# A chunked delta-rule attention with two dense blocks behind it: the 16 by 16 blocks inverted by 8 by 8 halves, and the key-scale steps split between odd and even chunks

## The chip, the core and the metric

The kernel runs on one core of one Trainium2 chip. The core has TensorE (PE, matmuls; PEld are its weight loads), VectorE (DVE), ScalarE (ACT), GpSimd (POOL) and SyncE (SP), which only issues transfers. Each engine works through its own list of instructions in order and waits on semaphores for the others. The metric is the device time in microseconds (us) of one execution; lower is better.

## The reference, cut to what matters

Inputs are q, k and v of shape (4, 8, 768, 48) and beta of shape (4, 8, 768), all float32. For each of the 32 pairs of batch and head:

```python
k_n = k / (np.linalg.norm(k, axis=-1, keepdims=True) + 1e-06)
for t in range(S):                       # S = 768
    y[t] = q[t] @ state                  # state is 48 x 48, zero at the start
    v_old = k_n[t] @ state
    state = state + beta[t] * outer(k_n[t], v[t] - v_old)
```

The result goes as x of shape (4, 768, 384) through two dense blocks: a Fourier transform over tokens and features, a layer norm and an MLP; then a gate by cosine and sine of x @ w_theta, a mix over tokens and one more layer. The change doesn't touch them.

## The kernel before

**Chunks.** The 768 steps are cut into 12 chunks of C = 64 tokens, numbered c = 0 to 11. Partitions hold two sets of 64 tokens (batches in halves), so NG = 16 groups stand beside each other on the free axis. Within a chunk the sequential rule is a triangular system. Its strictly triangular matrix comes from key products (`gram`). Its four 16 by 16 diagonal blocks (BLK = 16) are inverted exactly by DVE, all 128 of them at once, one a partition. What is left between the blocks is applied by three more matrix steps on PE (`hop` 1 to 3).

**What each engine does in iteration c.** All five engines run a loop `for c in range(-3, 12)`; the negative ones fill the pipeline.

- PE: `predicted(c)` (L360, keys times state), `corner(c, 0)` and `corner(c, 1)` (L305, operands TT and AP), `solve(c)` (L305, Yv and TT), `gram(c+2)` in two parts (L337), `hop` 1, 2, 3 (L305, Yv and ET), `turn(c+3)` (L325) before hop 3, `queried` (L394), `grow` (L420), `direct` (L305, Yv and AP).
- ACT copies what PE leaves in its banks: Yv after `solve` and after each hop (`copied_y(c, 0..3)`), AP after `gram`, KQ after `turn`, the state Sv, TT, the output Yo. It also makes the upper part of the diagonal blocks (Dy), and in odd iterations the square root of the key norms (`root`, nr<-nr). All of these are recorded as L443.
- DVE: `make_x(c)` (L672, Yv, v minus what the state predicts), `mask_e` (L660, ET), then for the next chunk `eliminate` (L630 and L633), `scaled_u` (L643, Ux) and `blocks_out` (L652, To, a transpose). Then, in odd iterations, `norm` (L563, sums of squared keys for a pair of chunks), and in even iterations `scale` (L576 to L589, eleven small steps that turn the norms into 1/norm and beta/norm²; ms and cT are results). Then `blocks_in(c+2)` (L603 Dy, L607 Tt, L614 Rb, L616 Ti, L618 and L620 U in bank 3).
- POOL: in odd iterations `squares` (L270, kk), then `scaled_v(c+1)` (L278, Vv by ms) and `mask_p(c+2)` (L290, AP). SP issues the loads of k, q and v.

**The inversion.** For a column j = 1 to 14 `eliminate` makes an outer product of U[0:j, j] and Ti[j, j+1:16] (L630) and subtracts it from U[0:j, j+1:16] (L633). Each of the 28 instructions waits for the one before. U lies in bank 3 (PSUM), Ti and prod in SBUF. ET, which `hop` 1 needs, and Yv, which `solve` needs, come before it in DVE's list.

**Order.** The lists are written out by hand as the loops have them. The semaphores that matter below: `solve` waits for both halves of Yv (s_xe) and for TT (s_tt); `corner` for TT and AP; `root` for both sums of its pair (s_n2) and for all steps of the pair before; `scale` for the root (s_sq); `blocks_in(n)` for the eleven steps of its pair (s_nr); `scaled_v` for the first five.

Of the kernel before, what the change touches and what calls it, by code (L numbers as in the profile page):

```python
# [8 lines left out]
ALU = mybir.AluOpType  # L9
ACT = mybir.ActivationFunctionType  # L10
AX = mybir.AxisListType
# [4 lines left out]
P = 128  # L16
# [11 lines left out]
BLK = 16  # L28
# [18 lines left out]
def constants():  # L47

    m, n = np.arange(HALF), np.arange(HALF + 1)
# [6 lines left out]
    d, k = np.arange(DM // 4 + 1), np.arange(DM // 4 + 1)  # L56
# [8 lines left out]
    p = np.arange(P)  # L65
    t, col = p % C, np.arange(C)
    mE = -1.0 * (t[:, None] // BLK < col[None, :] // BLK)
    mirrored = np.where(col == 0, 0, C - col)
    mP = 1.0 * np.stack([t[:, None] < col[None, :], t[:, None] < mirrored[None, :]], 1)
    upper = -1.0 * (np.arange(BLK)[:, None] < np.arange(BLK)[None, :])  # L70
    mU = np.broadcast_to(upper.reshape(1, BLK * BLK), (P, BLK * BLK))
# [15 lines left out]
def attention(nc, A, X, bank, block, sem, ident, preload, weights_ahead):  # L87
    with ExitStack() as ph:
        def sb(name, shape, dt=F32):
            return ph.enter_context(nc.sbuf_tensor(name, shape, dt))  # L90

        HG = NG // 2
        RK, RT, RA = 6, 4, 3
        half = (slice(0, C), slice(C, P))
        feat = (slice(0, D), slice(C, C + D))
# [24 lines left out]
        Rb = sb("Rb", [P, BLK, BLK])  # L120
        Ti = sb("Ti", [P, BLK, BLK])
        prod = sb("prod", [P, 56])
        Kb = sb("Kb", [P, RK, HG, 2, C])
        kk = sb("kk", [P, 2, NG, D])
        Vv = sb("Vv", [P, 2, NG, D])
        U = bank[3][:, 0:BLK * BLK].rearrange("p (k i) -> p k i", k=BLK)

        s_cst, s_id = sem("tables_loaded"), sem("identity_loaded")
# [20 lines left out]
        def there(n):  # L149
            return 0 <= n < NC  # L150
# [53 lines left out]

        STEPS = 2 + 28
        IN = 5
        NS = 11
# [233 lines left out]
        def _(act):  # L441
# [95 lines left out]
            for c in range(C0, NC):  # L537
                copied_y(c, 0)
                gram(c + 2, (0, 2))
                copied_y(c, 1)  # L540
                gram(c + 2, (1, 3))
                upper_blocks(c + 2)
                copied_y(c, 2)
                turned(c + 3)
                copied_y(c, 3)
                grown(c)
                placed(c + 1)
                output(c, 0)
                output(c, 1)
                if c % 2:  # L550
                    root((c + 3) // 2)
                store(c)

        @block.vector
        def _(dve):
# [8 lines left out]

            def scale(pair):
                if not 0 <= pair < NC // 2:
                    return
                dve.wait_ge(s_sq, pair + 1)
                if pair >= 2:
                    dve.wait_ge(s_vp, 2 * pair - 2)  # L570
                if pair >= 2:
                    dve.wait_ge(s_us, 2 * (2 * pair - 2))
# [18 lines left out]
                ]  # L591
                for i, step in enumerate(steps):
                    step().then_inc(s_nr, 1)
                    if i < NS - 1:
                        dve.wait_ge(s_nr, NS * pair + i + 1)

            def blocks_in(n):
# [17 lines left out]
                dve.wait_ge(s_in, at + 4)  # L615
                dve.tensor_tensor(Ti[:], Rb[:], by, ALU.mult).then_inc(s_in, 1)  # L616
                dve.wait_ge(s_in, at + 5)
                dve.tensor_tensor(bank[3][:, 0:BLK * BLK], Ti[:].rearrange("p j i -> p (j i)"), mU[:], ALU.mult).then_inc(s_iv, 1)  # L618
                dve.wait_ge(s_iv, STEPS * n + 1)
                dve.memset(bank[3][:, 0:BLK * BLK:BLK + 1], 1.0).then_inc(s_iv, 1)  # L620

            def eliminate(n, cols):
                if not there(n):
                    return
                for j in cols:
                    at = STEPS * n + 2 * j
                    m = BLK - 1 - j
# [1185 lines left out]
```

## Time and profile before

| | us |
|---|---|
| median of 3 runs | 832.17 |
| lowest, highest | 830.99, 832.19 |
| the profiled execution | 828.37 |
| its span | 826.6 |
| busy: PE, PEld | 776.2, 548.5 |
| busy: DVE, ACT, POOL | 517.9, 318.0, 164.7 |

The span is the stretch that the trace covers, from the first recorded work to the last; the 1.77 us between it and the time of the same execution lie around it. The profiled execution was 3.8 us faster than the median of the other runs, so sums made in the trace are compared with its own time and then carried over to the median. The attention part ends at 262.8 us of the span; the rest is the two dense blocks. A row of a timeline gives start, duration, engine, line, operation, the tiles out<-in with their shapes, the number of instructions, and in brackets the idle time before them with what ended it.

### The profile page before, as it was taken

The page shows a single profiled execution, that of the slowest core. Times are in us where ns is not written, and L with a number is a line of the kernel's source. Part 1 is how long each engine was busy: PE and PEld are TensorE (multiplying, and loading weights), DVE is VectorE, ACT ScalarE, POOL GpSimd, SP SyncE. Part 2 cuts the span into 40 slices and gives each one's busy share as a digit, 9 for nine tenths or more (in the row PEclk, how much of TensorE's full clock was granted, in tenths as well). Part 3 has the DMA queues.
Part 4 walks back from the last instruction along what each step waited for, and adds up shares of the span by engine and source line. Part 5 has one row for each costly group of instructions (what it writes and reads, how often), then busy time and mean ns, then how long its engine had stood idle before and what let it go on. Part 6 is the DMA issues. An engine that isn't in the chain of part 4 may idle for free.

```text
span 826.6 us, 24886 instructions
## 1 busy us (share of the span) xinstructions
PE 776.2 (94%) x10976; PEld 548.5 (66%) x10976; DVE 517.9 (63%) x1238; ACT 318.0 (38%) x635; POOL 164.7 (20%) x201
## 2 busy tenths in 40 slices
PE   4688888889889999999999999999999999999998
PEld 3687888888887556655665566666666666666664
DVE  4997889797847783724472346365646767767422
ACT  3465565655542350403140315142433434424211
POOL 2531423232200102200130010003213323224100
PEclk9899999999999999999999999999999999999999
DMA  9133343322121141010101001000000000000101
GB/s 210 41 92 82 94 110 91 90 71 62 42 80 42 58 131 41 12 47 1 41 18 58 1 29 29 1 1 1 1 1 1 11 20 20 36 14 20 39 28 50
DMA packets 45390, 37.54 MB, mean 45 GB/s; under 512 B 27425, under 2 KB 39651, under 8 KB 45283
## 3 DMA queue, kind: packets, MB, share of 16 engines
q1 hardware_dynamic: 38501, 30.90, 13.2%
q10 hardware_dynamic: 6781, 5.05, 2.5%
q8 instruction: 87, 1.43, 0.7%
q14 instruction: 21, 0.16, 0.1%
HBM read 26.50 MB, written 4.72 MB: 38 GB/s over the span
## 4 chain that ended last, share of the span: by engine, by line
PE 85%; DVE 5%; issue 4%; ACT 3%; DMA 2%; SPq 0%; POOL 0%; DVEq 0%; ACTq 0%
PE bank L305 15%; PE bank L1083 6%; PE bank L1131 6%; PE bank L1085 6%; PE bank L1130 6%; PE bank L1129 6%; PE bank L1084 6%; PE bank L1065 5%; PE bank L1067 5%; PE bank L1066 5%; PE bank L337 3%; PE bank L360 1%; ACT Dy L443 1%; PE bank L1107 1%; PE bank L1108 1%
## 5 line engine op out<-in xcount | busy, mean ns | idle before, releaser
L1248 ACT ACTIVATE hT_hi<-bank 128x384 f16<-128x384 f32 x96 | 46.7, 490 | 159.7 <-PE bank L1067 159.6
L1528 DVE SCALAR_TENSOR_TENSOR hT_lo<-bank,hT_hi 128x384 f16<-128x384 f32 x96 | 53.3, 556 | 73.3 <-ACT hT_hi L1248 72.5
L1065 PE MATMUL bank<-unT,wA 128*128 128x384 f16 x288 | 94.0, 326 | 0.3 <-DVE hT_lo L1528 0.3
L1083 PE MATMUL bank<-wA,hT_hi 128*128 128x384 f16 x288 | 93.9, 326 | 0.0
L1067 PE MATMUL bank<-unT,wA 128*128 128x384 f16 x288 | 93.9, 326 | 0.0
L1085 PE MATMUL bank<-wA,hT_lo 128*128 128x384 f16 x288 | 93.9, 326 | 0.0
L1066 PE MATMUL bank<-unT,wA 128*128 128x384 f16 x288 | 93.9, 326 | 0.0
L1084 PE MATMUL bank<-wA,hT_hi 128*128 128x384 f16 x288 | 93.9, 326 | 0.0
L305 PE MATMUL bank<-Yv,ET 64*64 64x48 f32 x2304 | 75.4, 218 | 4.2 <-ACT Yv L443 2.3
L305 PEld LDWEIGHTS bank<-Yv,ET 64*64 64x64 f32 x2304 | 72.9, 135 | 7.1 <-ACT Yv L443 4.5
L443 ACT ACTIVATE Yv<-bank,rows 128x384 f32<-128x384 f32 x72 | 40.6, 578 | 65.6 <-PE bank L305 65.4
L290 POOL TENSOR_TENSOR AP<-AP,mP 128x256 f32<-128x256 f32 x48 | 33.9, 728 | 141.4 <-ACT AP L443 132.1
L1536 DVE SCALAR_TENSOR_TENSOR X<-bank,X 128x384 f32<-128x384 f32 x24 | 13.4, 557 | 73.4 <-PE bank L1085 73.4
L955 POOL TENSOR_SCALAR fourier_temps<-fourier_temps 128x384 f32<-128x384 f32 x24 | 20.1, 837 | 153.2 <-DVE fourier_temps L1563 153.2
L1129 PE MATMUL bank<-wt_hi,z_first 128*128 128x384 f16 x144 | 46.9, 326 | 0.0
L1130 PE MATMUL bank<-wt_lo,z_first 128*128 128x384 f16 x144 | 46.9, 326 | 0.0
L1131 PE MATMUL bank<-wt_hi,z_first 128*128 128x384 f16 x144 | 46.9, 326 | 0.0
L1129 PE MATMUL bank<-wt_hi,wA 128*128 128x384 f16 x144 | 46.9, 326 | 0.0
L1130 PE MATMUL bank<-wt_lo,wA 128*128 128x384 f16 x144 | 46.9, 326 | 0.0
L1131 PE MATMUL bank<-wt_hi,wA 128*128 128x384 f16 x144 | 46.9, 326 | 0.0
L1065 PEld LDWEIGHTS bank<-unT,wA 128*128 128x128 f16 x288 | 28.2, 98 | 20.7 <-issue 1.8
L1066 PEld LDWEIGHTS bank<-unT,wA 128*128 128x128 f16 x288 | 28.2, 98 | 18.7 <-issue 1.1
(212 smaller groups left out, 1660.5 us busy)
## 6 DMA issues: line engine op xcount, KB each, us to landing
Kb<-k_dram SPq DMA_DIRECT2D x24, 192.0 KB, 3.6
Vv<-v_dram SPq DMA_DIRECT2D x12, 384.0 KB, 4.0
z_first<-w_dram SPq DMA_DIRECT2D x8, 576.0 KB, 4.0
z_first<-wt_dram SPq DMA_DIRECT2D x8, 576.0 KB, 3.6
out_dram<-hT_hi SPq DMA_DIRECT2D x24, 192.0 KB, 1.9
KQ<-q_dram SPq DMA_DIRECT2D x44, 96.0 KB, 2.3
X<-Yo ACTq DMA_DIRECT2D x12, 192.0 KB
X<-Yo ACTq DMA_DIRECT2D x10, 189.0 KB
```

Of the source, the lines that this page charges most:

```text
L305: mm = pe.matmul(out[half[h]], a[half[h]], b[half[h]], start=first, stop=last, skip_group_check=True)
L443: return nc.scalar.activation(out, in_, func, scale=scale)
L1065: pe.matmul(out, w1[0][:, k, cols], unT[0][:, k, :], start=(k == 0), stop=False)
L1066: pe.matmul(out, w1[0][:, k, cols], unT[1][:, k, :], start=False, stop=False)
L1067: mm = pe.matmul(out, w1[1][:, k, cols], unT[0][:, k, :], start=False, stop=(k == KD - 1))
L1083: pe.matmul(out, hT[0][:, f, cols], w2[0][:, f, :], start=(f == 0), stop=False)
L1084: pe.matmul(out, hT[0][:, f, cols], w2[1][:, f, :], start=False, stop=False)
L1085: mm = pe.matmul(out, hT[1][:, f, cols], w2[0][:, f, :], start=False, stop=(f == KF - 1))
L1129: pe.matmul(out, zh, wt[0][:, c, t, cols], start=first, stop=False)
L1130: pe.matmul(out, zh, wt[1][:, c, t, cols], start=False, stop=False)
L1131: mm = pe.matmul(out, zl, wt[0][:, c, t, cols], start=False, stop=last)
L1528: dve.scalar_tensor_tensor(hT[1][:, f, :], bank[3 + m % 3][:, 0:TG * P], 0.0, hT[0][:, f, :], ALU.max, ALU.subtract).then_inc(s_hl, 1)
```

## The change

The elimination now runs on the two 8 by 8 diagonal halves of each block at once, for columns 1 to 6 only, with a fourth axis of 2 in each access. The upper right 8 by 8 corner is then made by `corner_block`: a product of 512 elements (U's upper left half with Ti's corner), a sum over 8, a product of 512 with U's lower right half, and a sum over 8. Ti is now the negated block, so that its sign fits both. Of the eleven steps of `scale`, from pair 2 on the first five stand at the end of the odd iteration before, and the last six where all eleven stood. For this, in odd iterations from 1 on, `norm` moves up between the elimination and `corner_block`, and `root` on ACT moves from behind the output copies to ahead of `copied_y(c, 3)`. In iterations -3 to 0 the old places are kept.

```diff
-    upper = -1.0 * (np.arange(BLK)[:, None] < np.arange(BLK)[None, :])
+    upper = 1.0 * (np.arange(BLK)[:, None] < np.arange(BLK)[None, :])
...
+        def both_diagonal(padded):
+            t = padded.rearrange("p (b w) -> p b w", b=2)[:, :, 0:HB * BLK]
+            return t.rearrange("p b (k i) -> p b k i", k=HB)[:, :, :, 0:HB]
+
+        Ud, Td = both_diagonal(bank[3][:, 0:BLK * BLK + BLK]), both_diagonal(Ti_padded[:])
...
-        STEPS = 2 + 28
+        STEPS = 2 + 2 * (HB - 2) + 4
...
                 turned(c + 3)
+                if c % 2 and c > -1:
+                    root((c + 3) // 2)
                 copied_y(c, 3)
...
-                if c % 2:
+                if c in (-3, -1):
                     root((c + 3) // 2)
...
-                dve.wait_ge(s_sq, pair + 1)
-                if pair >= 2:
-                    dve.wait_ge(s_vp, 2 * pair - 2)
-                if pair >= 2:
+                if 0 in part:
+                    dve.wait_ge(s_sq, pair + 1)
+                    if pair >= 2:
+                        dve.wait_ge(s_vp, 2 * pair - 2)
+                elif pair >= 2:
                     dve.wait_ge(s_us, 2 * (2 * pair - 2))
...
-                dve.tensor_tensor(Ti[:], Rb[:], by, ALU.mult).then_inc(s_in, 1)
+                dve.scalar_tensor_tensor(Ti, Rb[:], -1.0, by, ALU.mult, ALU.mult).then_inc(s_in, 1)
...
-                    pr = prod[:, 0:j * m].rearrange("p (k i) -> p k i", k=j)
-                    dve.tensor_tensor(pr, U[:, 0:j, j:j + 1].broadcast_to([P, j, m]),
-                                      Ti[:, j:j + 1, j + 1:BLK].broadcast_to([P, j, m]), ALU.mult).then_inc(s_iv, 1)
+                    pr = prod[:, 0:2 * j * m].rearrange("p (b k i) -> p b k i", b=2, k=j)
+                    dve.tensor_tensor(pr, Ud[:, :, 0:j, j:j + 1].broadcast_to([P, 2, j, m]),
+                                      Td[:, :, j:j + 1, j + 1:HB].broadcast_to([P, 2, j, m]), ALU.mult).then_inc(s_iv, 1)
                     dve.wait_ge(s_iv, at + 1)
-                    dve.tensor_tensor(U[:, 0:j, j + 1:BLK], U[:, 0:j, j + 1:BLK], pr, ALU.subtract).then_inc(s_iv, 1)
+                    dve.tensor_tensor(Ud[:, :, 0:j, j + 1:HB], Ud[:, :, 0:j, j + 1:HB], pr, ALU.add).then_inc(s_iv, 1)
+
+            def corner_block(n):
...
+                dve.tensor_tensor(pr, U[:, 0:HB, 0:HB].unsqueeze(2).broadcast_to([P, HB, HB, HB]),
+                                  Ti[:, 0:HB, HB:BLK].rearrange("p l i -> p i l").unsqueeze(1).broadcast_to([P, HB, HB, HB]),
+                                  ALU.mult).then_inc(s_iv, 1)
+                dve.wait_ge(s_iv, at + 1)
+                dve.tensor_reduce(Xb[:], pr, AX.X, ALU.add).then_inc(s_iv, 1)
+                dve.wait_ge(s_iv, at + 2)
+                dve.tensor_tensor(pr, Xb[:].unsqueeze(2).broadcast_to([P, HB, HB, HB]),
+                                  U[:, HB:BLK, HB:BLK].rearrange("p l i -> p i l").unsqueeze(1).broadcast_to([P, HB, HB, HB]),
+                                  ALU.mult).then_inc(s_iv, 1)
+                dve.wait_ge(s_iv, at + 3)
+                dve.tensor_reduce(U[:, 0:HB, HB:BLK], pr, AX.X, ALU.add).then_inc(s_iv, 1)
...
-                eliminate(c + 1, (1, 2, 3, 4, 5, 6, 7, 8, 9, 10, 11, 12, 13, 14))
+                eliminate(c + 1, (1, 2, 3, 4, 5, 6))
+                if c % 2 and c > -1:
+                    norm((c + 3) // 2)
+                corner_block(c + 1)
                 scaled_u(c + 1)
                 blocks_out(c + 1)
-                if c % 2:
+                if c in (-3, -1):
                     norm((c + 3) // 2)
-                else:
-                    scale((c + 2) // 2)
+                elif c in (-2, 0):
+                    scale((c + 2) // 2, range(5))
+                if c % 2 and c > -1:
+                    scale((c + 3) // 2, range(5))
+                elif c % 2 == 0:
+                    scale((c + 2) // 2, range(5, NS))
                 blocks_in(c + 2)
```

On DVE, in the odd iteration 1, this is what stood between the last step of the elimination and the Yv of the next chunk before the change:

```order
L633 TENSOR_TENSOR bank<-bank,prod 128x14
L643 SCALAR_TENSOR_TENSOR Ux<-bank,rows,cT 128x16x16 x2
L652 STREAM_TRANSPOSE To<-Ux 128x16x32
L563 TENSOR_REDUCE nr<-kk 128x16 x2
L603 SCALAR_TENSOR_TENSOR Dy<-AP,rows,Dy 128x256 x2
L607 STREAM_TRANSPOSE Tt<-Dy 128x512
```

And this is what stands there now, from the last step of the shorter elimination on (prod and Xb are scratch tiles, bank is bank 3 with U in it):

```order
L645 TENSOR_TENSOR bank<-bank,prod 128x2x6
L574 TENSOR_REDUCE nr<-kk 128x16 x2
L653 TENSOR_TENSOR prod<-bank,Ti 128x512
L657 TENSOR_REDUCE Xb<-prod 128x64
L659 TENSOR_TENSOR prod<-Xb,bank 128x512
L663 TENSOR_REDUCE bank<-prod 128x8x8
L673 SCALAR_TENSOR_TENSOR Ux<-bank,rows,cT 128x16x16 x2
L682 STREAM_TRANSPOSE To<-Ux 128x16x32
L588 TENSOR_SCALAR nr<-nr 128x32
L589 RECIPROCAL nr<-nr 128x32
L590 TENSOR_TENSOR nr<-nr 128x32
L591 TENSOR_TENSOR nr<-nr 128x32
```

The two sums of squares have moved ahead of Ux, four instructions of the corner have come in, and the first scale steps (with L592, the fifth) have come in behind To; Dy follows them as before.

In the even iteration 2 the steps between To and Dy are now only these six:

```order
L682 STREAM_TRANSPOSE To<-Ux 128x16x32
L593 TENSOR_TENSOR nr<-ms 128x32
L594 RECIPROCAL nr<-nr 128x32
L595 TENSOR_TENSOR cd<-nr,bt 128x64
L599 STREAM_TRANSPOSE cx<-cd 128x64
L600 TENSOR_SCALAR cT<-cx,rows 128x32
L601 SCALAR_TENSOR_TENSOR cT<-cx,rows,cT 128x32
L615 SCALAR_TENSOR_TENSOR Dy<-AP,rows,Dy 128x256 x2
```

Before, the five steps L576 to L580 stood ahead of them.

On ACT in the odd iteration 1 the root (nr<-nr) stood behind the output copies Yo, with the stores behind it; now it stands ahead of the last copies of Yv:

```order
L452 ACTIVATE KQ<-bank 128x2x256 x2
L452 ACTIVATE nr<-nr 128x32
L452 ACTIVATE Yv<-bank 128x384 x2
L452 ACTIVATE Sv<-bank 128x384 x2
L452 ACTIVATE TT<-To,rows 128x16x32 x2
L452 ACTIVATE Yo<-bank 128x384 x2
L534 DMA X<-Yo 64x4x192 x2
```

So the copies of Yv, the state and TT now stand behind an instruction that waits for DVE's two sums.

## Rows read from the trace of the kernel before

**Rows 1.** Who waited for whom on PE from 60 to 240 us: total, times, longest.

```profile
PE bank L305 <- issue: 10.9, 14, 1.2
PE bank L360 <- issue: 4.3, 5, 0.9
PE bank L305 <- ACT Yv L443: 2.3, 5, 1.3
PE bank L420 <- issue: 2.2, 4, 0.6
PE bank L337 <- issue: 1.0, 2, 0.7
```

**Rows 2.** The same list for DVE, 60 to 240 us.

```profile
DVE Yv L672 <- PE bank L360: 18.0, 7, 4.7
```

**Rows 3.** Timeline of PE, iteration 5: predicted, corner, solve.

```profile
130.14 1.09 PE L360 MATMUL bank<-Sv,KQ 48*64 48x48 f32 x60
...
131.09 1.73 PE L305 MATMUL bank<-TT,AP 64*64 64x64 f32 x51
...
134.11 1.96 PE L305 MATMUL bank<-Yv,TT 64*64 64x48 f32 x62
```

**Rows 4.** Timeline of DVE, end of iteration 4, iteration 5, start of 6.

```profile
132.31 1.02 DVE L672 TENSOR_TENSOR Yv<-Vv,bank 128x384 f32<-128x384 f32 x2
...
134.94 0.16 DVE L630 TENSOR_TENSOR prod<-bank,Ti 128x14 f32<-128x14 f32 x1
...
143.83 1.74 DVE L563 TENSOR_REDUCE nr<-kk 128x16 f32<-128x768 f32 x2
...
152.12 1.02 DVE L672 TENSOR_TENSOR Yv<-Vv,bank 128x384 f32<-128x384 f32 x2 [3.10 <-PE bank L360]
```

**Rows 5.** Timeline of ACT, iteration 5: last copies of Yv, and the root.

```profile
145.41 0.52 ACT L443 ACTIVATE Yv<-bank 128x384 f32<-128x384 f32 x1
146.27 0.49 ACT L443 ACTIVATE Yv<-bank 128x384 f32<-128x384 f32 x1 [0.34 <-PE bank L305]
...
151.44 0.22 ACT L443 ACTIVATE nr<-nr 128x32 f32<-128x32 f32 x1
```

**Rows 6.** Timeline of DVE in the fill of the pipeline: elimination of chunk 0 onward.

```profile
20.23 0.17 DVE L630 TENSOR_TENSOR prod<-bank,Ti 128x14 f32<-128x14 f32 x1
...
26.89 1.13 DVE L643 SCALAR_TENSOR_TENSOR Ux<-bank,rows,cT 128x256 f32<-128x256 f32 x2
...
28.95 1.75 DVE L563 TENSOR_REDUCE nr<-kk 128x16 f32<-128x768 f32 x2
...
32.64 0.71 DVE L607 STREAM_TRANSPOSE Tt<-Dy 128x512 f32<-128x512 f32 x1
...
34.79 0.35 DVE L674 COPY Yv<-Vv 128x384 f32<-128x384 f32 x1
```

**Rows 7.** DVE by line and form, 0 to 262 us: busy us, mean ns, idle before.

```profile
L660 DVE TENSOR_TENSOR ET<-bank,mE 128x512 f32<-128x512 f32 x24 | 16.3, 688 | 4.7 <-PE bank L305 4.3
L603 DVE SCALAR_TENSOR_TENSOR Dy<-AP,rows,Dy 128x256 f32<-128x256 f32 x24 | 15.8, 696 | 1.6 <-ACT Dy L443 1.6
L643 DVE SCALAR_TENSOR_TENSOR Ux<-bank,rows,cT 128x256 f32<-128x256 f32 x24 | 13.9, 658 | 0.4
...
L563 DVE TENSOR_REDUCE nr<-kk 128x16 f32<-128x768 f32 x12 | 10.6, 922 | 8.2 <-DMA mE<-mE_dram 6.7 <-POOL kk L270 1.5
...
L614 DVE TENSOR_TENSOR Rb<-Tt 128x256 f32<-128x256 f32 x12 | 5.1, 426 | 0.4
...
L633 DVE TENSOR_TENSOR bank<-bank,prod 128x26 f32<-128x26 f32 x24 | 4.6, 193 | 0.8
```

**Rows 8.** Timeline of all engines about 31 us.

```profile
30.17 1.47 POOL L278 TENSOR_TENSOR Vv<-Vv,ms 128x768 f32<-128x768 f32 x1
...
30.57 0.91 PE L305 MATMUL bank<-TT,AP 64*64 64x64 f32 x12 [5.76 <-issue]
30.62 1.41 DVE L603 SCALAR_TENSOR_TENSOR Dy<-AP,rows,Dy 128x256 f32<-128x256 f32 x1
```

More of the change, by code:

```diff
@@ L93, in attention @@
         RK, RT, RA = 6, 4, 3
+        HB = BLK // 2
         half = (slice(0, C), slice(C, P))
@@ L120, in attention @@
         Rb = sb("Rb", [P, BLK, BLK])
-        Ti = sb("Ti", [P, BLK, BLK])
-        prod = sb("prod", [P, 56])
+        Ti_padded = sb("Ti", [P, BLK * BLK + BLK])
+        Ti = Ti_padded[:, 0:BLK * BLK].rearrange("p (k i) -> p k i", k=BLK)
+        prod = sb("prod", [P, HB * HB * HB])
+        Xb = sb("Xb", [P, HB, HB])
         Kb = sb("Kb", [P, RK, HG, 2, C])
@@ L563, in norm, with scale @@
                     dve.tensor_reduce(nr[:, 0, m * NG:(m + 1) * NG], kk[:, m], AX.X, ALU.add).then_inc(s_n2, 1)
-            def scale(pair):
+            def scale(pair, part):
                 if not 0 <= pair < NC // 2:
                     return
-                dve.wait_ge(s_sq, pair + 1)
-                if pair >= 2:
-                    dve.wait_ge(s_vp, 2 * pair - 2)
-                if pair >= 2:
+                if 0 in part:
[3 more added lines that the diff above has]
+                elif pair >= 2:
                     dve.wait_ge(s_us, 2 * (2 * pair - 2))
@@ L591, in scale @@
                 ]
[L592 to L595, printed above, removed]
+                for i in part:
+                    if i:
+                        dve.wait_ge(s_nr, NS * pair + i)
+                    steps[i]().then_inc(s_nr, 1)
             def blocks_in(n):
@@ L615, in blocks_in @@
                 dve.wait_ge(s_in, at + 4)
-                dve.tensor_tensor(Ti[:], Rb[:], by, ALU.mult).then_inc(s_in, 1)
+                dve.scalar_tensor_tensor(Ti, Rb[:], -1.0, by, ALU.mult, ALU.mult).then_inc(s_in, 1)
                 dve.wait_ge(s_in, at + 5)
-                dve.tensor_tensor(bank[3][:, 0:BLK * BLK], Ti[:].rearrange("p j i -> p (j i)"), mU[:], ALU.mult).then_inc(s_iv, 1)
+                dve.tensor_tensor(bank[3][:, 0:BLK * BLK], Ti_padded[:, 0:BLK * BLK], mU[:], ALU.mult).then_inc(s_iv, 1)
                 dve.wait_ge(s_iv, STEPS * n + 1)
@@ L626, in eliminate @@
                     at = STEPS * n + 2 * j
-                    m = BLK - 1 - j
+                    m = HB - 1 - j
                     dve.wait_ge(s_iv, at)
-                    pr = prod[:, 0:j * m].rearrange("p (k i) -> p k i", k=j)
-                    dve.tensor_tensor(pr, U[:, 0:j, j:j + 1].broadcast_to([P, j, m]),
-                                      Ti[:, j:j + 1, j + 1:BLK].broadcast_to([P, j, m]), ALU.mult).then_inc(s_iv, 1)
+                    pr = prod[:, 0:2 * j * m].rearrange("p (b k i) -> p b k i", b=2, k=j)
+                    dve.tensor_tensor(pr, Ud[:, :, 0:j, j:j + 1].broadcast_to([P, 2, j, m]),
+                                      Td[:, :, j:j + 1, j + 1:HB].broadcast_to([P, 2, j, m]), ALU.mult).then_inc(s_iv, 1)
                     dve.wait_ge(s_iv, at + 1)
-                    dve.tensor_tensor(U[:, 0:j, j + 1:BLK], U[:, 0:j, j + 1:BLK], pr, ALU.subtract).then_inc(s_iv, 1)
+                    dve.tensor_tensor(Ud[:, :, 0:j, j + 1:HB], Ud[:, :, 0:j, j + 1:HB], pr, ALU.add).then_inc(s_iv, 1)
+            def corner_block(n):
+                if not there(n):
+                    return
+                at = STEPS * (n + 1) - 4
+                pr = prod[:].rearrange("p (k i l) -> p k i l", k=HB, i=HB)
+                dve.wait_ge(s_iv, at)
+                dve.tensor_tensor(pr, U[:, 0:HB, 0:HB].unsqueeze(2).broadcast_to([P, HB, HB, HB]),
[9 more added lines that the diff above has]
+                dve.tensor_reduce(U[:, 0:HB, HB:BLK], pr, AX.X, ALU.add).then_inc(s_iv, 1)
             def scaled_u(n):
```

## The prediction

> **What bounds the kernel now.** I read the page first: PE is busy in 94% of the span, and the change doesn't touch PE's work. It can help only where PE waits for DVE or for something that DVE releases. So the second view is the list of waits on PE over nine chunks, 60 to 240 us [rows 1]. PE stands idle for 20.7 us in 180, of which 18.4 are "issue" (PE waited for nothing that the profile shows) and 2.3 are for copies of Yv by ACT. No row names DVE. The counter-view is DVE's own list [rows 2]: seven times in these nine chunks DVE stood ready and waited for PE, 18.0 us in all.
>
> The third view is the timelines of one pair of chunks. `solve(5)` needs the first half of Yv and PE's own corner products. DVE's Yv starts at 132.31 with no idle time before it [rows 4], some 1.1 us after the matmuls of L360 that it needs, which run from 130.14 to 131.23 [rows 3]. So in this iteration, behind the even one with eleven scale steps, DVE is late. But PE has 64 corner matmuls to do meanwhile, from 131.09 on, and starts `solve` at 134.11 [rows 3]. The first half of Yv is there at 132.31 + 0.5 = 132.8 and the second at 133.3. The lateness is paid from a margin of 1.3 us. Behind the odd iteration DVE waited 3.10 us for PE, at 152.12 [rows 4].
>
> The exception is the fill of the pipeline. Nothing else runs there, and DVE works without a pause from the elimination of chunk 0 at 20.23 to the first Yv at 34.79 [rows 6]. Each microsecond saved in that chain can move everything behind it.
>
> **The inversion.** Before, the 28 steps of chunk 0 take 26.89 − 20.23 = 6.66 us [rows 6]. After, twelve steps of 12 to 24 elements and four of 512 elements stand there.
> - The small ones: an instruction of 26 elements takes 193 ns and leaves 0.8 us idle before 24 of them, 0.03 each [rows 7]. A pair costs 2 × 0.22 = 0.45, six pairs 2.7 us. A fourth axis in the access is not in the trace; I take it as free, since sizes, not axes, move these durations.
> - The two sums over 512 elements: the sum over 768 takes 922 ns [rows 7]. The slope from 426 ns (256 elements, contiguous) to 688 ns (512) is 1.02 ns an element, so a sum of 512 takes about 922 − 256 × 1.02 = 660 ns, two of them 1.3 us.
> - The two products of 512 elements: one operand of each steps by 16 elements. The lower bound is the contiguous 512 of ET, 0.69 us each. The nearest rows are those with a stepped operand: Ux takes 658 and Dy 696 ns for 256 elements against 426 for Rb [rows 7], so the step costs 0.23 to 0.27 us for 256 and twice that for 512. That gives 1.15 to 1.23; I take 1.2 each. As the upper bound the penalty counts twice (both inputs): 0.69 + 1.08 = 1.77 each.
> - The corner is then 2.4 + 1.3 + 4 × 0.03 = 3.8 us (2.8 to 5.0), and the whole inversion 6.5 us (5.5 to 7.7) against 6.66. The saving is 0.2 us a chunk, between 1.2 saved and 1.0 lost. Sixteen fewer instructions nearly buy back to what there was, because 2048 elements come in.
>
> The Trainium skill ("Vector Engine (DVE) Microarchitecture Reference", section 5.2) has a rule on this: a port keeps full rate only for runs of two adjacent words, one source that hops every element runs at 1.73 ns an element, and small steps at about 2.5. Our stepped rows come out at about 2 ns, between the two. By 1.73 the saving would be some 0.5 us, by 2.5 it would be a loss of about 0.3.
>
> **What becomes of it in the fill.** The chain behind the inversion of chunk 0 is Ux, To, the sums, Dy, Tt, and on to Yv. Before, the first Dy starts at 30.62 and takes 1.41 us where the mean is 0.70 [rows 7, 8]. It lies beside POOL's scaling of V, 30.17 to 31.64, and ends 0.39 us after it. POOL's work there hangs on the start of the elimination, not on its end, so it stays where it is. If Dy starts 0.2 us earlier it still ends at 32.03: the saving goes into a longer Dy, and Tt (32.64), Yv (34.79) and `solve(0)` don't move. Only with 0.45 us saved or more does Dy start ahead of 30.17; then the second Dy lies beside POOL instead, and about 0.6 us is gained. With 1.2 us both Dy are through, and some 1.7 us is gained. A loss is swallowed in the same way up to about 0.4 us. My value is therefore 0, with 0 to 1.7 us gained from the lower bounds, and about 0.5 us lost from the upper one.
>
> The Trainium skill ("SBUF — State Buffer", "Who interferes with whom") says that a DVE instruction with two SBUF inputs contends with a GpSimd instruction that reads SBUF. The trace agrees: Dy has two such inputs and stretches, while Ux (one input in PSUM) takes its usual 1.13 us for two.
>
> **The scale steps, in chunks 1 to 7.** The five steps that move are worth 1.1 us of small work, more where POOL runs beside them. The even iteration gets shorter by them, the odd one longer by the same. DVE's lateness before odd chunks (1.1 us in chunk 5) turns into a wait for PE, and the wait of 3.10 us before even chunks falls to 1.5 to 2 us. Neither is on the path: 0. The queue that this concerns is DVE's; behind the steps stand Dy to U of the next chunk and then Yv. The four roots: scale step 1 now waits for a root that comes after the KQ copies, about 145.6 in iteration 5, and To ends near 139.4 + 3.8 (corner) + 1.1 (Ux) + 1.0 (To) = 145.3, so DVE waits some 0.3 us, covered by the same slack.
>
> **The root and the sums.** In iteration 5 the elimination starts at 134.94 [rows 4]. With 2.7 us for the small steps and 1.74 for the two sums, `root` is free at about 139.4. ACT comes to it at 145.4, 6 us later. Its 0.22 us delay the first copy of Yv, which started without idle time at 145.41; the second one waited 0.34 us for PE [rows 5], and `grow` needs both. The root fits into that pause: 0. If the cover is gone it costs 0.2 us in each of four odd chunks, 0.8 us.
>
> **The sum.** Chunk 0's inversion 0 (−1.7 to +0.5), the eleven others 0, scale 0, root 0 (to +0.8). The dense blocks only shift. The profiled execution's 828.37 stays about there, say 828.2 with a small share of the early-Dy case; the median stands 3.8 us above it, and 832.17 − 0.2 gives 832.0. What a measurement of this kernel can tell from no change is 0.2%, 1.7 us.
>
> **Rivals.**
> 1. The stepped operands cost less than Ux and Dy say, and in the fill both Dy pass ahead of POOL: 830.4 to 831.6. For it: the products write contiguously, where Ux and Dy also write with a step. Against: Dy also reads with one. The far end just passes the bound. Chance 0.13.
> 2. The lateness of DVE does reach PE in the chunks, and "issue" hides it. DVE showed no wait before Yv in two of nine chunks in rows 2; with about 1 us in each of the four even-to-odd passages and the fill, 832.2 − 5 = 827. Against it: the waits of PE fall inside runs of one kind of matmul, and not at `solve`. Chance 0.06.
> 3. Slower: `root` holds ACT. The norm of a pair is late (its squares by POOL, or the key load), ACT stands at `root` in iterations 1, 3, 5 and 7, and the copies of Yv, `grow`, Sv and the next `predicted` wait behind. It decides only when the sums end over 6 us later than I work out. With 1 us of holding each it would be 832.2 + 4 = 836. Chance 0.03.
> 4. The corner costs its upper bound, 1.0 us more than it removes. The fill loses 0.5. In iteration 0, which keeps all eleven steps, Yv(1) is late by 1 us with little margin left. Together 1.5 us: 833.7. Chance 0.06.
> 5. Nothing moves, as forecast: 832.0, its own range 830.8 to 833.0. Chance 0.72.
>
> **Numbers.** Faster by over 0.2%: rival 2 with 0.06, half of rival 1, and a share of what the trace can't show, 0.14. Slower: rival 3 and part of rival 4, 0.07. The rest, 0.79, is no change. The range of 829.8 to 833.7 takes in rivals 1 and 4 and leaves out 2 and 3.
>
> **What would show it.** In the profile after: the two products at about 1.2 us and the sums at 0.66; the inversion of chunk 0 at about 6.5 us; a first Dy stretched past 1.41 us with Tt still near 32.6 and Yv near 34.8; DVE waiting for PE before nearly all Yv, no row with DVE in PE's list; the root ahead of the last copies of Yv without a wait for the sums; PE idle about as long as before. I am wrong if `solve(0)` starts over 1 us earlier, if the steady chunks get shorter than before, or if ACT waits for L574.

## The result and the profile after

| | before | after |
|---|---|---|
| median of 20 runs each, us | 832.92 | 836.86 |
| lowest, highest | 827.68, 838.75 | 830.27, 840.41 |
| ratio of the runs | | 1.0036 [1.0020, 1.0053] |
| profiled execution, its span | 828.37, 826.6 | 837.56, 835.7 |

The change makes the kernel 0.36% slower, 3.0 us by the ratio, with an interval of 0.20 to 0.53% (the two medians lie 3.9 us apart). The forecast was 832.0, no change. Single runs of one kernel lie up to 11 us apart: the three runs that the prediction had (830.99 to 832.19) showed far too little of that. The two profiled executions lie at different places in this spread, so their 9 us difference can't be put down to the change. Only what stands in a fixed place of both traces is compared below, and each such place is looked for in the traces of the experiments.

**The steady chunks went as forecast.** Waits of PE from 60 to 240 us after the change (engine, tile, line, what it waited for: total, times, longest), against [rows 1]:

```profile
PE bank L314 <- issue: 14.3, 17, 1.5
PE bank L369 <- issue: 3.8, 5, 0.9
PE bank L314 <- ACT Yv L452: 2.2, 4, 1.3
PE bank L429 <- issue: 1.9, 4, 0.8
PE bank L346 <- issue: 1.0, 3, 0.6
PE bank L334 <- issue: 0.4, 1, 0.4
```

No row names DVE, and Yv costs what it did. "Issue" is 21.4 us where it was 18.4. The same sum is 22.0 in a second trace of the kernel before (experiment 1), so these 3 us don't speak against the change. The list of DVE, same stretch, against [rows 2]:

```profile
DVE Yv L702 <- PE bank L369: 24.1, 9, 4.4
DVE ET L690 <- PE bank L314: 4.5, 6, 1.4
DVE nr L588 <- ACT nr L452: 2.4, 4, 0.7
```

DVE now waits nine times in nine chunks for PE before Yv, not seven times. In iteration 5 the rows are these (start, duration, and in brackets the idle time before):

```profile
135.53 1.02 DVE L702 TENSOR_TENSOR Yv<-Vv,bank 128x384 f32<-128x384 f32 x2 [2.62 <-PE bank L369]
...
149.29 0.18 DVE L588 TENSOR_SCALAR nr<-nr 128x32 f32<-128x32 f32 x1 [0.63 <-ACT nr L452]
...
156.47 1.02 DVE L702 TENSOR_TENSOR Yv<-Vv,bank 128x384 f32<-128x384 f32 x2 [2.49 <-PE bank L369]
```

The 0.63 us for the root (0.7 at most, forecast 0.3) sit inside the slack: at its next Yv DVE still waits 2.49 us for PE. Behind even iterations, where it was late, there are 2.62 us of slack now.

ACT in iteration 5, against [rows 5]:

```profile
148.06 1.09 ACT L452 ACTIVATE KQ<-bank 128x512 f32<-128x512 f32 x2
149.03 0.23 ACT L452 ACTIVATE nr<-nr 128x32 f32<-128x32 f32 x1
149.57 0.49 ACT L452 ACTIVATE Yv<-bank 128x384 f32<-128x384 f32 x1 [0.31 <-PE bank L314]
150.50 0.49 ACT L452 ACTIVATE Yv<-bank 128x384 f32<-128x384 f32 x1 [0.44 <-PE bank L314]
```

The root follows the copies of KQ without a pause, and both copies of Yv behind it still wait for PE. It costs nothing.

**The fill didn't.** DVE from its first loads to the first Yv after the change, against [rows 6]:

```profile
9.56 0.95 DVE L574 TENSOR_REDUCE nr<-kk 128x16 f32<-128x768 f32 x1 [7.88 <-DMA mE<-mE_dram]
...
13.19 0.95 DVE L574 TENSOR_REDUCE nr<-kk 128x16 f32<-128x768 f32 x1 [2.68 <-POOL kk L279]
...
22.46 0.07 DVE L632 MEMSET bank<- 128x16 f32 x1
...
22.57 0.17 DVE L642 TENSOR_TENSOR prod<-bank,Ti 128x12 f32<-128x12 f32 x1
...
25.15 1.04 DVE L653 TENSOR_TENSOR prod<-bank,Ti 128x512 f32<-128x512 f32 x1
26.23 0.69 DVE L657 TENSOR_REDUCE Xb<-prod 128x64 f32<-128x512 f32 x1
26.95 0.69 DVE L659 TENSOR_TENSOR prod<-Xb,bank 128x512 f32<-128x512 f32 x1
27.67 0.69 DVE L663 TENSOR_REDUCE bank<-prod 128x64 f32<-128x512 f32 x1
28.40 1.14 DVE L673 SCALAR_TENSOR_TENSOR Ux<-bank,rows,cT 128x256 f32<-128x256 f32 x2
...
32.14 2.79 DVE L615 SCALAR_TENSOR_TENSOR Dy<-AP,rows,Dy 128x256 f32<-128x256 f32 x2
34.96 0.71 DVE L619 STREAM_TRANSPOSE Tt<-Dy 128x512 f32<-128x512 f32 x1
...
37.12 0.35 DVE L704 COPY Yv<-Vv 128x384 f32<-128x384 f32 x1
...
37.61 2.72 PE L314 MATMUL bank<-Yv,TT 64*64 64x48 f32 x62 [2.03 <-DVE Yv L704]
```

And the same kinds of instruction before the change, where [rows 6] begin only later:

```profile
8.38 0.95 DVE L563 TENSOR_REDUCE nr<-kk 128x16 f32<-128x768 f32 x1 [6.71 <-DMA mE<-mE_dram]
...
10.87 0.95 DVE L563 TENSOR_REDUCE nr<-kk 128x16 f32<-128x768 f32 x1 [1.53 <-POOL kk L270]
...
20.13 0.07 DVE L620 MEMSET bank<- 128x16 f32 x1
...
35.29 2.01 PE L305 MATMUL bank<-Yv,TT 64*64 64x48 f32 x62 [1.04 <-DVE Yv L674]
```

The inversion of chunk 0 begins with the setting of U's diagonal (the memset), at 22.46 and before at 20.13: 2.33 us late *before the first step of the elimination has run*. From there on to Tt it is 12.50 us, before 12.51. So the first Yv is late by 37.12 − 34.79 = 2.33 us, all of it from ahead of the elimination, and PE, which waits for it, starts `solve(0)` at 37.61 in place of 35.29. The second sum of squares is late by 2.32; it waits for POOL's squares of keys, and these for the loads of k. The view of DMA says why. From 0 to 24 us, for the kernel before, the queue that carries the loads (packets, MB, time of its packets as a share of 16 engines) and the loads into Kb (median us from issue to landing):

```profile
q1 hardware_dynamic: 11632, 3.71, 68.2%
...
Kb<-k_dram SPq DMA_DIRECT2D x10, 192.0 KB, 3.8
```

The same for the changed kernel:

```profile
q1 hardware_dynamic: 11632, 3.71, 92.9%
...
Kb<-k_dram SPq DMA_DIRECT2D x10, 192.0 KB, 5.3
```

As many packets and bytes take 36% more of the queue's time. The key loads consist of packets of 192 bytes (one token's 48 features); of those that start in the first 20 us such a packet takes 15.6 ns on average before and 22.2 ns after. Loads into other tiles, which share the 16 DMA engines, are later too: `ident` lands 6.1 us after its issue, before 4.8. Nothing in the change touches a load. What it touches is the list of tiles: Ti grows by 64 bytes a partition, prod from 224 to 2048, and Xb adds 256. They stand ahead of Kb (k), kk (its squares) and Vv (v), so Kb starts at byte 184,928 of each partition where it stood at 182,784, 2144 further.

### The profile page after: what moved, and what is told of

Read it like the earlier page. It is cut to its first block, busy times and chain, and to the rows that moved or that the text cites. A ratio compares the mean times of both kernels' runs of the same rounds, so it can differ in the third digit from the quotient of the medians.

```text
span 835.7 us, 24746 instructions
## 1 busy us (share of the span) xinstructions
PE 779.0 (93%) x10976; PEld 550.5 (66%) x10976; DVE 516.6 (62%) x1094; ACT 318.4 (38%) x635; POOL 166.1 (20%) x201
## 3 DMA queue, kind: packets, MB, share of 16 engines
q8 instruction: 87, 1.43, 0.7%
## 4 chain that ended last, share of the span: by engine, by line
PE 85%; DVE 5%; issue 4%; ACT 3%; DMA 2%; SPq 1%; POOL 0%; DVEq 0%; ACTq 0%
PE bank L314 15%; PE bank L1120 6%; PE bank L1168 6%; PE bank L1167 6%; PE bank L1122 6%; PE bank L1166 6%; PE bank L1121 6%; PE bank L1102 5%; PE bank L1104 5%; PE bank L1103 5%; PE bank L346 3%; PE bank L369 1%; PE bank L1144 1%; PE bank L1145 1%; PE bank L1143 1%
```

## The experiments

All ratios are of times against the kernel before on the same chip, with 95% intervals. Five theories are named in the expectations. A: DVE, being earlier, moves the loads of V, which then collide with the transfers of PE's instructions. B: the root holds ACT. C: chance only. D: the tiles' alignment to 64 bytes is lost (184,928 is a multiple of 32 only), later widened to D2: the place of a tile in SBUF, whatever the alignment. E: the number of DVE's instructions moves where its code is fetched. Two numbers of each trace tell most: the mean 192-byte packet of the first 20 us, and the start of the first Yv.

**Runs 1 to 4: the kernel before, each part of the change alone, the change once more.** Run 1 has no edit and run 4 is the changed kernel. Run 2 takes the halves, with `norm`, `scale` and `root` where they were (both cuts are against the kernel before):

```diff
-        STEPS = 2 + 28
+        STEPS = 2 + 2 * (HB - 2) + 4
...
-                eliminate(c + 1, (1, 2, 3, 4, 5, 6, 7, 8, 9, 10, 11, 12, 13, 14))
+                eliminate(c + 1, (1, 2, 3, 4, 5, 6))
+                corner_block(c + 1)
```

Run 3 keeps the old elimination and takes the rest:

```diff
+                if c % 2 and c > -1:
+                    root((c + 3) // 2)
                 copied_y(c, 3)
...
-                eliminate(c + 1, (1, 2, 3, 4, 5, 6, 7, 8, 9, 10, 11, 12, 13, 14))
+                eliminate(c + 1, (1, 2, 3, 4, 5, 6))
+                if c % 2 and c > -1:
+                    norm((c + 3) // 2)
+                eliminate(c + 1, (7, 8, 9, 10, 11, 12, 13, 14))
...
```

> The kernel before, unchanged, as a measure of what differs between two traces of one program. All theories: ratio 1.000 within its interval. The theory of collisions (A: DVE is earlier, so the load of V, which waits for Yv, starts earlier against PE's stream and delays PE's own instruction transfers) and the theory of luck (C: the stretches marked issue vary from execution to execution and nothing else is there) both expect the issue time of PE from the first Yv to the last to vary; C expects a spread of 3 us or more between two traces, A one of under 2.

> The inversion by halves alone, scale steps, norm and root where they were. The shorter inversion makes DVE 0.8 us earlier in each chunk. A (collisions) expects a part of the loss, 1 to 2 us (ratio 1.001 to 1.002). Theory B (the root ahead of the last Yv copies holds ACT) expects 1.000. C expects 1.000.

> The scale steps split, norm and root moved, the inversion over 14 columns as before. A expects most of the loss, 2 to 3 us (1.002 to 1.004), since DVE's lateness in odd iterations goes. B expects all of it, 3 us (1.0036). C expects 1.000.

> The changed kernel once more, beside the others on the same chip. A and B: 1.0036 again, within 1.002 to 1.005. C: as likely 1.000.

| run | ratio | packet, ns | first Yv, us |
|---|---|---|---|
| 1 before again | 1.0016 [0.9995, 1.0037] | 15.6 | 35.18 |
| 2 halves only | 1.0043 [1.0021, 1.0065] | 22.6 | 37.02 |
| 3 split only | 1.0022 [1.0003, 1.0041] | 15.5 | 34.55 |
| 4 after again | 1.0054 [1.0031, 1.0077] | 22.7 | 37.32 |

The slowness comes with the halves: run 2 has it with the root where it was, so B can't be the cause of it, and it comes back in run 4, which chance alone doesn't explain. Run 3 doesn't settle B by itself: its interval begins just above 1 and would hold the 1.0036 that B expected, and it can't be told from run 1 either. The slow key loads are in both traces with the halves and in neither of the others. From the first to the last Yv it is 220.4 us in run 1, and 214.1 in the first trace of the same program: a trace's chunks can't be compared to better than 6 us.

**Runs 5 to 8: alignment.** Run 5 adds `pad = sb("pad", [P, 8])` behind Xb (Kb at 184,960, a multiple of 64 again), run 7 the same to run 2's kernel, run 8 puts the pad ahead of all tiles instead. Run 6 takes the kernel before and shifts Kb by 32 bytes:

```diff
-        prod = sb("prod", [P, 56])
+        prod = sb("prod", [P, 64])
```

> The changed kernel with an unused tile of 32 bytes a partition behind Xb, so that Kb, kk and Vv start at a multiple of 64 bytes again, as before the change (they start 32 bytes off one in the changed kernel, since prod, Ti and Xb grew by 2144 bytes). Theory D (placement: packets of 192 bytes into a row 32 bytes off a multiple of 64 take longer, 22.2 ns against 15.6 in the first 20 us, which delays the first keys and PE's own instruction transfers): the loss goes, ratio 1.000 (0.998 to 1.002), packets back at 15.6 ns, first Yv near 34.8 us. A (DVE is earlier) and B (root): ratio stays at 1.004.

> The kernel before with prod of 64 in place of 56 floats, which puts Kb, kk and Vv 32 bytes off a multiple of 64; no instruction changes. D: all of the loss appears, ratio 1.004 (1.002 to 1.006), packets at 22 ns in the first 20 us, first Yv near 37 us. A and B: 1.000.

> The inversion by halves alone, with the same 32 bytes behind Xb. D: 1.000, against 1.0043 without them. A: 1.001 to 1.002, B: 1.000 in both.

> The changed kernel with 32 unused bytes ahead of ident instead, so that Kb and Vv, but also ident, KQ, Yo, the first weights and bt start at a multiple of 64 bytes, which they don't in either kernel. D: 1.000 or lower; rows of 2048 and 3072 bytes are longer than those of keys, so they gain less by it: 0 to 2 us below the first of these runs (0.997 to 1.000). A and B: 1.004.

| run | ratio | packet, ns | first Yv, us |
|---|---|---|---|
| 5 after, aligned | 1.0021 [0.9995, 1.0047] | 22.6 | 36.92 |
| 6 before, shifted | 0.9992 [0.9969, 1.0016] | 15.4 | 34.88 |
| 7 halves, aligned | 1.0037 [1.0013, 1.0061] | 22.2 | 36.59 |
| 8 after, all aligned | 1.0018 [0.9994, 1.0042] | 22.6 | 36.25 |

D falls from both sides, by the packets: aligned again, they stay slow, and misaligned they stay fast. The ratios of runs 5 and 8 alone, whose intervals hold 1, couldn't have said so.

**Runs 9 to 12: length of the code, or place of the tiles.** Runs 9 (changed) and 10 (before) get 140 one-word memsets on DVE in the dense blocks, which brings it to 1410 and 1550 instructions:

```diff
+        filler = sb("filler", [P, 140])
...
+                if m < 70:
+                    for i in range(2):
+                        dve.memset(filler[:, 2 * m + i:2 * m + i + 1], 0.0)
```

Run 11 is the kernel before with `prod` widened from 56 to 600 elements that nothing uses: Kb, kk and Vv stand 2176 bytes further, near their place after the change, and no instruction differs. Run 12 is the changed kernel, all its instructions as they are, with the large scratch tiles behind the loaded ones, so that Kb, kk and Vv stand where they stood before:

```diff
-        prod = sb("prod", [P, HB * HB * HB])
-        Xb = sb("Xb", [P, HB, HB])
+        gap = sb("gap", [P, 40])
         Kb = sb("Kb", [P, RK, HG, 2, C])
         kk = sb("kk", [P, 2, NG, D])
         Vv = sb("Vv", [P, 2, NG, D])
+        prod = sb("prod", [P, HB * HB * HB])
+        Xb = sb("Xb", [P, HB, HB])
```

> The changed kernel with 140 memsets of one word on DVE in the MLP (two behind each of 70 makings of hT_lo, where DVE waits 0.76 us each time), so that DVE's program has the 1410 instructions it had before the change (1270 now). Theory E (length of the program: with a shorter program something of the load, as the place of inputs in HBM, differs, the first loads run slower, 22 ns a key packet against 15.6, and the fill ends 2.2 us later): packets back at 15.6 ns, first Yv near 34.8 us, ratio 1.000 to 1.002. Theory D2 (place of the tiles in SBUF): 22 ns and 37 us as before, ratio 1.003 to 1.005.

> The kernel before with the same 140 memsets (1550 instructions on DVE). E: the first loads may change either way, so 15.6 or 22 ns; at 22 ns the ratio is 1.003. D2: 15.6 ns, 34.8 us, ratio 1.000 (the memsets lie in DVE's waits).

> The kernel before with prod of 600 in place of 56 floats: no instruction changes, Kb, kk and Vv lie 2176 bytes higher, where the changed kernel has them within 32 bytes. D2: 22 ns a key packet in the first 20 us, first Yv near 37 us, ratio 1.003. E: 15.6 ns, 34.8 us, 1.000.

> The changed kernel with prod and Xb placed behind Vv, so that Kb, kk and Vv have the very addresses of before. D2: 15.6 ns, 34.8 us, ratio 1.000 to 1.002. E: 22 ns, 37 us, 1.003 to 1.005.

| run | ratio | packet, ns | first Yv, us |
|---|---|---|---|
| 9 after, filled | 1.0019 [0.9997, 1.0042] | 22.6 | 36.79 |
| 10 before, filled | 1.0003 [0.9982, 1.0023] | 15.4 | 34.81 |
| 11 before, far | 1.0018 [0.9995, 1.0040] | 22.6 | 36.52 |
| 12 after, near | 1.0000 [0.9983, 1.0018] | 15.5 | 34.35 |

E falls: the packets keep their side whatever the number of instructions. Runs 11 and 12 are the pair that decides on the fill. The kernel before with its tiles moved, 0 to 24 us:

```profile
q1 hardware_dynamic: 11632, 3.71, 92.2%
...
Kb<-k_dram SPq DMA_DIRECT2D x10, 192.0 KB, 5.0
```

The changed kernel with its tiles moved back, same stretch:

```profile
q1 hardware_dynamic: 11632, 3.71, 68.2%
...
Kb<-k_dram SPq DMA_DIRECT2D x10, 192.0 KB, 3.9
```

The share of the queue changes sides with the place of the tiles, whatever the instructions. Both halves of the difference are there: 92 to 93% far, 68% near. The time of run 12 is that of the kernel before, to 0.18%: placed like this, the change does what was forecast of it, nothing. It has all the instructions of the changed kernel, with DVE as early, so A falls by it too.

**Runs 13, 14 and 17: which tile, and how far.** Run 13 puts a gap of 2176 bytes between Kb and kk (Kb stays, kk and Vv move). Runs 14 and 17 are the kernel before with `prod` at 328 and 1080 elements, Kb moved by 1088 and 4096 bytes:

```diff
         Kb = sb("Kb", [P, RK, HG, 2, C])
+        gap = sb("gap", [P, 544])
```

> The kernel before with 2176 unused bytes between Kb and kk: Kb keeps its address, kk and Vv lie 2176 bytes higher. If the place of Kb is what makes the first loads slow: 15.6 ns a key packet in the first 20 us, ratio 1.000. If that of Vv: 22 ns, first Yv near 37 us, 1.002 to 1.003.

> The kernel before with prod of 328 floats, so that Kb, kk and Vv lie 1088 bytes higher, half of the way. If the slowness sets in at a boundary, 15.6 or 22.5 ns tells on which side of 1088 bytes it lies; if it grows with the distance, about 19 ns.

> The kernel before with prod of 1080 floats: Kb, kk and Vv lie 4096 bytes higher, one slot of Kb. If the first loads slow down above some address of Kb (between 1088 and 2144 bytes above the old one): 22 ns a key packet, first Yv near 37 us, ratio 1.002 to 1.003. If it goes by the address within a slot of 4096 bytes, which is the old one here: 15.6 ns, 34.8 us, 1.000.

| run | ratio | packet, ns | first Yv, us |
|---|---|---|---|
| 13 kk and Vv far | 0.9999 [0.9974, 1.0024] | 15.6 | 35.25 |
| 14 moved by 1088 | 1.0004 [0.9980, 1.0028] | 15.5 | 34.55 |
| 17 moved by 4096 | 1.0010 [0.9987, 1.0033] | 15.6 | 34.42 |

Run 17, the furthest of all, 0 to 24 us:

```profile
q1 hardware_dynamic: 11632, 3.71, 69.1%
...
Kb<-k_dram SPq DMA_DIRECT2D x10, 192.0 KB, 4.1
```

So it goes with Kb's place; moving kk and V alone does nothing (Kb alone was never moved). Nor is it a border in the partition that the whole tile has crossed: it is slow 2144 and 2176 bytes up and fast 0, 32, 1088 and 4096 up. A slot of Kb takes 4096 bytes; within a slot Kb starts at byte 608 or 640 where the packets are slow, and at 2560, 2592 or 3648 where they aren't.

All of these starts fit one simple reading. In Kb the 48 floats of each key row start at a multiple of 256 bytes from the tile's start. Kb's own start leaves a remainder by 256 of 0, 32 or 64 in the kernels with 15 to 16 ns a packet, where a packet of 192 bytes ends at or before the next multiple of 256, and of 96 or 128 in those with 22 ns, where every packet runs across it. (Multiples of 64 or 128 don't tell them apart: every packet crosses one at every place.) No run was made to test this, for instance with Kb only 96 bytes up, and what in the memory or the DMA engines would make it so wasn't tried.

**Runs 15, 16 and 18: keep POOL out of Dy's way.** With the tiles near, two Dy of the fill still take 2.51 us, beside POOL's scaling of V. Run 15 (to run 12) and run 16 (to the kernel before) make POOL wait for DVE's first store into U of chunk 1:

```diff
+                if c == 0:
+                    pool.wait_ge(s_iv, STEPS + 1)
```

Run 18 is run 15 with `pool.wait_ge(s_xe, 2)`, the end of the first Yv.

> The changed kernel with Kb, kk and Vv at their old addresses, and in iteration 0 POOL waits for the first store into U of chunk 1 before it scales V of chunk 1, so that this no longer lies beside DVE's Dy in the fill. If the saving of the inversion went into a Dy that POOL stretched: the two Dy take 1.3 us in place of 2.8, first Yv at 32.9 in place of 34.4 us, ratio 0.998 (0.996 to 1.000). If not: as e12_after_near, 1.000.

> The kernel before with the same wait on POOL. By the same reason the two Dy take 1.3 us in place of 2.0, first Yv at 34.1, ratio 0.999; without it 1.000.

> As e15_near_apart, but POOL's scaling of V of chunk 1 waits for both copies of Yv of chunk 0 in place of the store into U: there it lay beside the second copy, which took 1.62 us against 0.35. The second copy back at 0.35 us, solve of chunk 0 without a pause between its halves, 0.6 to 1.2 us less than e15: ratio 0.997 (0.995 to 0.999). If the fill no longer sets the time: 0.9976 as e15.

| run | ratio | two Dy, us | U's memset | first Yv |
|---|---|---|---|---|
| 12, for comparison | 1.0000 [0.9983, 1.0018] | 2.51 | 20.00 | 34.35 |
| 15 near, apart | 0.9976 [0.9955, 0.9998] | 1.37 | 19.77 | 33.00 |
| 16 before, apart | 0.9987 [0.9966, 1.0008] | 1.22 | 19.84 | 33.74 |
| 18 near, apart, late | 0.9993 [0.9977, 1.0010] | 1.36 | 20.14 | 33.37 |

DVE of run 12:

```profile
20.00 0.07 DVE L633 MEMSET bank<- 128x16 f32 x1
...
29.66 2.51 DVE L616 SCALAR_TENSOR_TENSOR Dy<-AP,rows,Dy 128x256 f32<-128x256 f32 x2
...
34.35 0.35 DVE L705 COPY Yv<-Vv 128x384 f32<-128x384 f32 x1
```

And of run 15, with POOL's scaling of V where it is now:

```profile
29.44 1.37 DVE L618 SCALAR_TENSOR_TENSOR Dy<-AP,rows,Dy 128x256 f32<-128x256 f32 x2
...
33.00 0.35 DVE L707 COPY Yv<-Vv 128x384 f32<-128x384 f32 x1
...
33.02 1.65 POOL L288 TENSOR_TENSOR Vv<-Vv,ms 128x768 f32<-128x768 f32 x1 [3.17 <-DVE bank L633]
...
33.26 1.62 DVE L707 COPY Yv<-Vv 128x384 f32<-128x384 f32 x1
```

Dy takes half, and from U's memset to the first Yv it is 13.23 us in place of 14.35: the 1.1 us are gained where the prediction saw them. With the old inversion (run 16) the same stretch is 13.90 us, before 14.66, so once POOL is away the halves are worth 0.67 us of their 0.83. In run 15 the second copy of Yv then meets POOL (1.62 us for 0.35); run 18 moves POOL behind it and that copy is back at 0.35. Run 18 gains in its trace, but its time can't be told from that of the kernel before, and the 0.997 that was expected of it isn't there; run 15's interval lies just below 1. Together they stand at about 0.9985, so I don't call any version faster than the kernel before.

**The runs taken together.** Eight measurements have Kb at a place with 22 ns a packet (the changed kernel, runs 2, 4, 5, 7, 8, 9, 11); the mean of their ratios is 1.0031, and their first Yv starts at 36.25 to 37.32 us. Eight runs have it at a place with 15 to 16 ns and POOL where it was (1, 3, 6, 10, 12, 13, 14, 17): mean 1.0006, first Yv at 34.35 to 35.25. The difference is 0.25%, 2.1 us, as much as the fill shows. The ratios share runs of the kernel before and single ones don't settle it (run 11's interval holds 1). Seven of the first eight also have the new inversion, so the two comparisons that change the place alone count most. They are made from the single times of the chip on which runs 9 to 12 were timed (means, 95% by resampling): with the old instructions run 11 is 1.5 us [0.4, 2.7] above the kernel before and run 10, with the new ones run 9 is 2.2 us [0.6, 3.7] above run 12. With the place kept, run 12 differs from the kernel before and run 10 by −0.2 us [−1.3, 0.7].

## Why the prediction was wrong, point by point

**The step that failed** is a term that the sum doesn't have. The section on the fill takes the start of the elimination of chunk 0, 20.23 us, as given: POOL's work hangs on it, the prediction says, "so it stays where it is". The change moved that start by 2.3 us, through the tiles it enlarges. The diff shows both (`prod` and `Xb` ahead of Kb), and [rows 6] and the prediction's own sentence, that each microsecond in this chain moves everything behind it, give the price: 832.2 + 2.3 = 834.5 by its own sum. How a tile's place could change a load no row of before showed. But of the five rivals only the third names a late key load, and there as something that holds ACT in the chunks, not as a start of the fill that moves, and the range ended at 833.7. Of the prediction's signs, "Tt still near 32.6 and Yv near 34.8" failed (34.96 and 37.12). The list under "I am wrong if" had an earlier `solve(0)`, but not a later one.

What is left, 3.0 us by the ratio against 2.3, lies within the interval of the ratio (1.7 to 4.4 us). Runs 2 and 4, at 1.0043 and 1.0054, leave room for a further loss in the chunks. Later 192-byte packets take 16.3 to 17.1 ns in kernels with Kb at such a place (2144 or 2176 bytes up) and 15.8 to 16.1 in the others, but the chunks of a single program differ by 6 us between traces, so whether this costs anything is open.

The granted clock is no better account of it. In the trace after, the clock is at its lower level just when `solve(0)` runs, and by the start of the second `hop` (44.72 us, before 40.83) the distance between the two traces has grown from 2.3 to 3.9 us. But run 12, with Kb at its old place, has a lower clock there as well (0.60 and 0.54 from 36 to 40 us), and runs 2 and 11, with Kb moved, don't (1.00 from 38 us on). With one trace of each kernel a small share of the clock's in the 3 us can't be excluded.

**What bounds the kernel**: right. PE's list still names no work of DVE's.

**The inversion of chunk 0**: 28.40 − 22.57 = 5.83 us, forecast 6.5, before 6.66. The small steps take 2.58 (forecast 2.7), the sums 0.69 each (0.66). The first product takes 1.04 (1.2) and the second only 0.69 (1.2): its operand that steps by 16 elements lies in PSUM and costs what a contiguous one does. The mis-sized term is that product's, by 0.5 us. The first one, with the stepped operand in SBUF, is 0.35 us above a contiguous product, where I had taken 0.5. By the rule of the Trainium skill ("Vector Engine (DVE) Microarchitecture Reference", section 5.2), 1.73 ns an element for one source that hops every element, the estimate is 0.69 + 512 × (1.73 − 1.05) = 1.04 us, 1.05 being its figure for contiguous ones, and the trace agrees. Its 2.5 ns for small steps would make it 1.43 us by the same estimate, and that the trace doesn't show. The prediction's "sixteen fewer instructions" was a slip: 28 become 16, twelve fewer in each inversion.

**What becomes of it in the fill**: the value of 0 was nearly right, its threshold not. 0.83 us were saved, and by the prediction's "0.45 us or more" 0.6 of it should have come through. From U's memset to Tt it is 12.50 and 12.51. With the whole chain 2.3 us later, POOL's work had moved along, and the first Dy takes 2.22 us. The two engines about 33 us after the change, against [rows 8]:

```profile
32.14 2.22 DVE L615 SCALAR_TENSOR_TENSOR Dy<-AP,rows,Dy 128x256 f32<-128x256 f32 x1
...
32.50 1.47 POOL L287 TENSOR_TENSOR Vv<-Vv,ms 128x768 f32<-128x768 f32 x1
```

Dy has started *ahead* of POOL and still ends 0.39 us behind it, at 34.36 and 33.97, as in [rows 8]. The prediction had let an instruction already under way pass. It does so in other traces. Run 12 about 31 us:

```profile
29.66 0.83 DVE L616 SCALAR_TENSOR_TENSOR Dy<-AP,rows,Dy 128x256 f32<-128x256 f32 x1
...
30.05 1.74 POOL L288 TENSOR_TENSOR Vv<-Vv,ms 128x768 f32<-128x768 f32 x1
...
30.41 1.75 DVE L616 SCALAR_TENSOR_TENSOR Dy<-AP,rows,Dy 128x256 f32<-128x256 f32 x1
```

Here the first Dy passes, POOL's instruction takes 1.74 us in place of 1.47, and the second Dy is held. Eight traces have the new inversion and POOL where it was. In each POOL starts 0.35 to 0.39 us behind the first Dy. In four (after, runs 2, 4, 5) it goes as in the first pair of rows and nothing is gained; in four (runs 7, 8, 9, 12) as in the second, and from U's memset to the first Yv it is 14.35 us in place of 14.67. So 0.3 us comes through or none, never the 0.6 of the prediction; what decides between the two is open. Only with POOL elsewhere (runs 15 and 18 against 16) do 0.67 us come through.

**The scale steps**: right. DVE waits before every Yv (2.49 us at the one behind iteration 5, forecast 1.5 to 2), and run 3 measures 1.0022 beside 1.0016 for the kernel before itself, though its interval, from 1.0003 to 1.0041, leaves room for a small loss.

**The root**: right in the trace of iteration 5. The wait for it is up to 0.7 us, and covered.

**Rivals.** Rival 2 (DVE's lateness reaches PE) would have made run 12 faster; it is 1.0000. Rival 3 (the root holds ACT) is excluded by the rows of ACT and by run 2, which is slow without it, rival 4 (the corner costs its upper bound) by 5.83 us. Rival 1 is half right: the operands are cheaper, but both Dy never passed ahead of POOL, and one of them only in four of eight traces. Rival 5 is what run 12 shows with the tiles in place: the forecast was one for the instructions, and the change was more than these.

## What to carry to other kernels

A change of a scratch tile's size moves every tile behind it: compare the addresses of the tiles that small-packet loads fill (by the reading above, whether a packet runs across a multiple of 256 bytes), and look at the packets' share of their queue in the first microseconds, before explaining a slower kernel by its instructions. A control with the old instructions and the new addresses, and its mirror image, tells the two apart in two runs. And where two engines contend for operands, don't count on starting ahead of the rival: here a lead of 0.4 us bought nothing in four traces and 0.3 us in four others, and moving the rival bought 0.7.

## What the runs showed of the hardware

- The place of a destination tile in SBUF sets how fast 192-byte packets go in the crowded first 20 us: 15.2 to 16.2 ns a packet in the eleven runs with Kb at or near its old place, 1088 or 4096 bytes up, and 22.2 to 22.7 ns in the seven runs and the changed kernel's trace with it 2144 to 2176 bytes up. Later packets into the same places differ by far less (16.3 to 17.1 against 15.8 to 16.1 ns). The shifts by 32 bytes that were tried did nothing. The places with 22 ns are those where a packet crosses a multiple of 256 bytes; that this is the cause wasn't tested.
- An operand of DVE that steps by 16 elements costs nothing where it lies in PSUM (a product of 512 elements in 0.69 us), and in SBUF half as much again (1.04 us).
- When POOL's scaling of V starts 0.35 to 0.39 us into DVE's Dy (0.70 us on average), either this Dy takes 2.2 us and POOL its usual 1.47 (four traces), or Dy takes 0.8, POOL 1.7 and the next Dy 1.75 (four traces). A copy takes 1.62 us for 0.35 beside an instruction of that kind (1.65 us in run 15).
- The granted clock falls to its lower level, 1.2 GHz, at different places in different executions of one program. In the trace after it does so at `solve(0)` and the `gram` behind it, after PE had been busy for 0.39 of 2 us, and PE is busy throughout while the clock is low (columns: window; length and PE, PEld, DVE, ACT, POOL busy; clock as a share of 2.4 GHz, DMA share, GB/s):

```profile
36.00:38.00 2.00, 0.39 (x13) 0.42 (x15) 1.87 (x7) 0.00 (x0) 0.00 (x0) 1.00 0.01 4
38.00:40.00 2.00, 2.00 (x55) 2.00 (x52) 1.83 (x8) 0.58 (x1) 0.00 (x0) 0.66 0.58 142
40.00:42.00 2.00, 2.00 (x44) 2.00 (x41) 1.76 (x8) 0.58 (x1) 0.00 (x0) 0.50 0.35 117
```

  The second trace of the changed kernel (run 4) has three more such stretches within the chunks, at 83, 107 and 209 us, and 228.2 us from first to last Yv where the first had 221.5. With such a spread the three runs at hand for the prediction couldn't show an effect of 0.3%, and with 10 to 12 runs of a kernel the interval of a ratio still reaches some 0.2% to either side.
